# The last block of a three-stage kernel in seven products, and a second phase with new places

## What is computed

```python
# attention, per head: state = gamma*state + k v^T ; y = scale * q state
x = attn_out.reshape(3072, 512)
h = x @ w_in                               # 512 -> 2048
g = where(h >= 1, h, where(h <= -1, 0, (h + 1)**2 / 4))
x = g @ w_out                              # 2048 -> 512
h = x @ w_in2                              # 512 -> 1024
solu = h * softmax(h)
ln = (solu - mean(solu)) / sqrt(var(solu) + 1e-6) * g_ln
out = ln @ w_out2                          # 1024 -> 512
```

## Time and profile before

| | |
|---|---|
| three runs | 850.82, 851.32, 851.6 us; median 851.32 |
| profiled execution | 851.47 us, of which the span of the trace is 849.7 us |
| PE busy | 842.8 us, 99% of the span |
| DVE, ACT, POOL busy | 65%, 42%, 35% |
| granted PE clock | full in all 40 slices of the span |

### The profile page before, as it was taken

The page is one execution under the profiler, slowest core; times in us unless marked ns, Lnnn a source line. Parts: engine busy times, 40 slices in busy tenths (PEclk is TensorE's granted clock), DMA queues, the critical chain, the costliest instruction groups (busy, mean ns, idle before and its releaser), DMA issues.

```text
span 849.7 us, 14124 instructions
## 1 busy us (share of the span) xinstructions
PE 842.8 (99%) x5392; PEld 718.7 (85%) x5392; DVE 548.8 (65%) x1020; ACT 356.0 (42%) x557; POOL 293.6 (35%) x278
## 2 busy tenths in 40 slices
PE   8999999999999999999999999999999999999998
PEld 7788888888888888888988888888887888888886
DVE  5556567766754575545854563566888898898831
ACT  3444342323322243223422233256566766675642
POOL 2687555445323253324322222236441112221000
PEclk9999999999999999999999999999999999999999
DMA  9934358864443435443443404200165554456351
GB/s 338 386 113 143 125 174 305 259 204 149 150 134 129 139 122 161 146 133 123 135 148 124 125 26 149 100 25 25 51 217 170 167 165 150 149 186 181 117 175 61
DMA packets 75588, 129.14 MB, mean 152 GB/s; under 512 B 7552, under 2 KB 25984, under 8 KB 75520
## 3 DMA queue, kind: packets, MB, share of 16 engines
q1 hardware_dynamic: 74944, 127.71, 46.0%
q10 hardware_dynamic: 576, 0.52, 0.2%
HBM read 94.65 MB, written 33.55 MB: 151 GB/s over the span
## 4 chain that ended last, share of the span: by engine, by line
PE 94%; DMA 2%; DVE 1%; SPq 1%; issue 1%; POOL 0%; ACT 0%; DVEq 0%
PE acc L646 31%; PE h L550 19%; PE o_ps L1448 14%; PE p L1348 11%; PE h L616 10%; PE att L493 3%; PE att L504 2%; PE att L528 1%; PE att L518 1%; DMA z<-zq 1%; DMA q<-in_q 1%; DMA x_raw<-x2T 1%; PE acc L504 0%; PE h L633 0%; SPq L322 0%
## 5 line engine op out<-in xcount | busy, mean ns | idle before, releaser
L646 PE MATMUL acc<-g_hi,w 128*128 128x512 f32 x768 | 258.7, 398 | 0.0
L1122 POOL TENSOR_TENSOR g_lo<-g_raw,g_hi 128x512 fp32r<-128x512 f32 x96 | 130.9, 1364 | 312.4 <-ACT g_hi L690 312.4
L646 PEld LDWEIGHTS acc<-g_hi,w 128*128 128x128 f32 x768 | 144.1, 188 | 35.7 <-issue 3.4
L760 ACT ACTIVATE g_raw<-g_raw,half_bias 128x512 f32<-128x512 f32 x96 | 69.2, 721 | 234.4 <-DVE g_raw L972 234.4
L985 DVE TENSOR_TENSOR h<-h 128x256 f32<-128x256 f32 x192 | 81.1, 423 | 110.5 <-PE h L550 79.4
L646 PE MATMUL acc<-g_lo,w 128*128 128x512 f32 x384 | 150.1, 391 | 0.0
L690 ACT ACTIVATE g_hi<-g_raw 128x512 fp32r<-128x512 f32 x96 | 60.7, 632 | 86.6 <-DVE g_raw L977 86.6
L550 PE MATMUL h<-x_hi,s 128*128 128x256 f32 x512 | 93.7, 281 | 0.0
L972 DVE TENSOR_SCALAR g_raw<-h 128x512 f32<-128x512 f32 x96 | 52.1, 543 | 61.4 <-PE acc L646 59.7
L977 DVE TENSOR_TENSOR g_raw<-h,g_raw 128x512 f32<-128x512 f32 x96 | 68.2, 710 | 23.9 <-ACT g_raw L760 23.9
L550 PEld LDWEIGHTS h<-x_hi,s 128*128 128x128 f32 x512 | 81.0, 189 | 2.4
(11 more groups left out here) (140 smaller groups left out, 1491.4 us busy)
## 6 DMA issues: line engine op xcount, KB each, us to landing
s<-w_sums SPq DMA_DIRECT2D x128, 256.0 KB, 2.8
z<-zq SPq DMA_DIRECT2D x24, 512.0 KB, 2.8
zt<-z SPq DMA_DIRECT2D x92, 128.0 KB, 3.1
kT<-in_kT SPq DMA_DIRECT2D x24, 256.0 KB, 3.1
q<-in_q SPq DMA_DIRECT2D x24, 256.0 KB, 2.8
v<-in_v SPq DMA_DIRECT2D x24, 256.0 KB, 3.2
w_sums<-s_made SPq DMA_DIRECT2D x6, 1024.0 KB, 5.1
x2T<-y SPq DMA_DIRECT2D x24, 256.0 KB, 3.3
```

What stands on the lines that cost most here:

```text
L646: last = mm(acc[m][:, :], ww, gg[:, f % 2, :], start=f == 0 and t == 0, stop=f == FT1 - 1 and t == 2)
L760: nc.scalar.activation(gate[:, f % 2, :], gate[:, f % 2, :], ACT.Square, bias=half_bias[:, 0:1], scale=0.5).then_inc(sem["squared"], 1)
L1122: tt(g[1][:, f % 2, :], gate[:, f % 2, :], g[0][:, f % 2, :].bitcast(F32), ALU.subtract)\
```

## The change

Block 5 becomes the fifth block in seven products, for its first 14 pieces (7 pairs, `WHOLE` = 14); pieces 14 and 15 stay one by one. The order at the end of block 5 on PE is: up 14, down 12, up 15, down 13, and then the second phase, whose first pair is now P1, P2, P6, P7, P4, P5, P3 with nothing between P7 and P4, followed by down 14 and 15. The sums of w2_in move from DVE to POOL (at pairs 2 and 3). The preparation of ACT and DVE moves to the ends of pairs 3 to 6 and to the new `last_steps`; the four last low parts of w2_out on DVE now stand before the joins of the first pair. ACT's high parts of the second piece of x2 (x2_1 and its sums) move behind `copy_part(0)`. In the last block x has eight parts, since b12 is needed beside t1, and t1 gets a place of its own. In the second phase P1 of the fourth pair (n = 3) is issued ahead of down product 2. Tiles of the second phase get new addresses.

```diff
-SEVEN = range(1, BLOCKS - 1)
-LAST_Q = FPAIRS * len(SEVEN)
+SEVEN = range(1, BLOCKS)
+LAST = BLOCKS - 1
+WHOLE = FT1 - 2
+LAST_Q = FPAIRS * (len(SEVEN) - 1) + WHOLE // 2
+def pairs(blk):
+    return range(WHOLE // 2 if blk == LAST else FPAIRS)
+X_ORDER = (("t3", "b11", "b21", "t2", "t1", "b22", "t4"), ("b11", "b21", "t3", "t2", "t1", "b22", "t4", "b12"))
...
# SP
+                    if blk == LAST and p == 4:
+                        load_w2_out()
...
+                    if blk == LAST and p == 0:
+                        load_w2_in()
...
-                sp.wait_ge(sem["g_used"], FT1 * (BLOCKS - 1) + 8 + 2 * n)
+                sp.wait_ge(sem["g_used"], FT1 * LAST + 10 + 2 * n)
...
# PE
-                for p in range(FPAIRS):
+                for p in pairs(blk):
                     pair(blk, p)
-            dense(BLOCKS - 1)
+            for f in range(WHOLE, FT1):
+                up(LAST, f)
+                down(LAST, f - LAG)
...
# ACT
+            def prepare(p):
+                for kt in {3: (0, 1), 4: (2, 3)}.get(p, ()):
+                    w2_in_high(kt)
+                if p == 5:
+                    for i in range(3):
+                        w2_sum_high(i)
+                for piece in {5: (0, 1), 6: (2, 3)}.get(p, ()):
+                    w2_out_high(piece)
+
+            def last_steps():
+                square(LAST, WHOLE - 1)
+                high(LAST, WHOLE - 1)
+                x2_high(0)
+                x2_sum_high(0)
+                square(LAST, WHOLE)
+                high(LAST, WHOLE)
+                for piece in (4, 5):
+                    w2_out_high(piece)
+                square(LAST, WHOLE + 1)
+                high(LAST, WHOLE + 1)
+                for piece in (6, 7):
+                    w2_out_high(piece)
...
# DVE
+            def prepare(p):
+                for kt in {4: (0, 1), 5: (2, 3)}.get(p, ()):
+                    w2_in_low(kt)
+                if p == 6:
+                    for i in range(2):
+                        w2_sum_low(i)
+
+            def last_steps():
+                dve.wait_ge(sem["taken1"], 7 * LAST_Q)
+                clamp(LAST, WHOLE - 1)
+                larger(LAST, WHOLE - 1)
+                w2_sum_low(2)
+                dve.wait_ge(sem["gains"], 16)
+                for piece in range(2):
+                    w2_out_lo(piece)
+                clamp(LAST, WHOLE)
+                x2_low(0, "x2_0")
+                larger(LAST, WHOLE)
+                x2_low(1, "x2_sum0")
+                for piece in range(2, 4):
+                    w2_out_lo(piece)
+                clamp(LAST, WHOLE + 1)
+                larger(LAST, WHOLE + 1)
...
# POOL, in pair(blk, p), behind low(blk, f)
+                if blk == LAST and p in (2, 3):
+                    sums_of_w2(p - 2)
+                if blk == LAST and p == 6:
+                    sums_of_x2(0)
...
+            def last_steps():
+                for f in range(WHOLE - 1, FT1):
+                    low(LAST, f)
+                    if f == WHOLE:
+                        sums_of_x2(1)
...
# second phase, PE
-                    finish["pe_down"](FT1 - LAG - 1)
-                    finish["pe_up"]()
                     pe.wait_ge(sem["taken"], 1)
                     p4()
...
-                    p1()
+                    if n > 3:
+                        p1()
...
                 for s in DOWNS.get(n, ()):
+                    if s == 2:
+                        up_first(3)
                     down(s)
...
# second phase, ACT
             copy_part(0)
-            finish["act_square"]()
-            finish["act_high"]()
+            x2_high(1)
+            x2_sum_high(1)
             exponential(0, SECOND)
...
# second phase, DVE
+            for piece in range(4, FT2):
+                finish["dve_w2_out"](piece)
             join_p2(0)
             join_p6(0)
             join_p7(0)
-            for piece in range(4, FT2):
-                finish["dve_w2_out"](piece)
-            finish["dve_clamp"]()
             join_p4(0)
-            finish["dve_larger"]()
             join_p5(0)
             join_p3(0)
```

More of the change, by code:

```diff
@@ L220, in place @@
         split_in_place(f"x2_sum{n}", [P, 4, 2, P])
-    assert cursor[0] <= w_at + 10 * 8192
+    assert cursor[0] <= w_at + 12 * 8192
+    for name in ("h2", "e"):
+        plain(name, [P, 2, FF2])
+    assert cursor[0] <= w_at + 14 * 8192
+    plain("zq", [P, 2, P // SQ, FT2, SQ])
+    assert cursor[0] <= w_at + 15 * 8192
+    plain("zt", [P, 2, P // SQ, FT2, SQ])
+    zT = [[put(f"zT{n}_{part}", [P, FT2, P], F32R) for part in ("hi", "lo")] for n in (1, 2)]
+    assert cursor[0] <= y_at
+    cursor[0] = x3_at
+    plain("solu", [P, 2, FF2])
+    split("zT0", [P, FT2, P])
+    mem["zT1"], mem["zT2"] = zT
     zT_hi4 = cursor[0]
     cursor[0] += P * FT2 * 4
[L224 to L232, removed]
+    assert cursor[0] <= w_pair_at
     cursor[0] = g_at
@@ L650, in dense @@
             def dense(blk):
-                for f in range(steps(blk)):
-                    if blk == 0 and f == 0:
+                for f in range(FT1):
+                    if f == 0:
                         first_up()
@@ L767, in dense @@
             def dense(blk):
-                if blk - 1 in SEVEN:
-                    square(blk - 1, FT1 - 1)
-                    high(blk - 1, FT1 - 1)
-                for f in range(steps(blk)):
-                    change = f == FT1 - 1 and blk + 1 == SEVEN[0]
-                    if f == FT1 - 2 and blk + 1 == SEVEN[0]:
+                for f in range(FT1):
+                    change = f == FT1 - 1
+                    if f == FT1 - 2:
                         split_part(blk + 1, "t3")
@@ L801, in pair @@
                 f = 2 * p
-                more = blk + 1 in SEVEN and p == FPAIRS - 1
-                last = blk + 1 not in SEVEN and p == FPAIRS - 1
+                more = blk < LAST and p == FPAIRS - 1
                 if p == 1:
@@ L837, in _ @@
             for blk in SEVEN:
-                for p in range(FPAIRS):
+                for p in pairs(blk):
                     pair(blk, p)
-            dense(BLOCKS - 1)
-            finish["act_square"] = lambda: square(BLOCKS - 1, FT1 - 1)
-            finish["act_high"] = lambda: high(BLOCKS - 1, FT1 - 1)
+            last_steps()
+            finish["act_x2"] = (x2_high, x2_sum_high)
             finish["act_evacuate"] = lambda: evacuate(BLOCKS - 1)
@@ L1033, in pair @@
                         sums_low(q + AHEAD, n)
+                if blk == LAST:
+                    prepare(p)
             def dense(blk):
-                if blk - 1 in SEVEN:
-                    dve.wait_ge(sem["taken1"], 7 * LAST_Q)
-                    clamp(blk - 1, FT1 - 1)
-                    larger(blk - 1, FT1 - 1)
-                for f in range(steps(blk)):
-                    change = f == FT1 - 1 and blk + 1 == SEVEN[0]
-                    if blk < BLOCKS - 1:
-                        attention(blk + 1, 2 * f)
-                    if f == LAG - 1 and blk:
-                        evacuate(blk - 1)
+                for f in range(FT1):
+                    change = f == FT1 - 1
+                    attention(blk + 1, 2 * f)
                     if change:
@@ L1081, in _ @@
             for blk in SEVEN:
-                for p in range(FPAIRS):
+                for p in pairs(blk):
                     pair(blk, p)
-            dense(BLOCKS - 1)
+            last_steps()
             finish["dve_w2_out"] = w2_out_lo
-            finish["dve_clamp"] = lambda: clamp(BLOCKS - 1, FT1 - 1)
-            finish["dve_larger"] = lambda: larger(BLOCKS - 1, FT1 - 1)
             finish["dve_evacuate"] = lambda: evacuate(BLOCKS - 1)
@@ new lines, in dense @@
+            def dense(blk):
+                for f in range(FT1):
+                    attention(blk + 1, 2 * f)
+                    attention(blk + 1, 2 * f + 1)
+                    for name in {FT1 - 3: ("t3",), FT1 - 2: ("t1", "t2", "t4")}.get(f, ()):
+                        sum_of_x(blk + 1, name)
+                    low(blk, f)
+                    for piece in w_out_at(f):
+                        split_weights(piece)
+                    if f in PREPARE_AT:
+                        sums_of_weights(PREPARE_AT.index(f))
@@ L1790, in _ @@
             finish["pool_x2_lo"](1)
-            finish["pool_low"]()
             root(0, SECOND)
```

387 lines of the change are left out of this document (181 added, 206 removed).

## The result

| | before | changed |
|---|---|---|
| median | 851.07 us (850.44 to 851.6, 4 runs) | 858.48 us (857.71 to 860.11, 4 runs) |
| profiled execution, span of its trace | 851.47, 849.7 | 858.88, 857.1 |
| granted PE clock over the span | 1.0 | 0.998 |

The changed kernel is slower: ratio 1.0085, 95% interval 1.0072 to 1.0097, or +7.4 us. The forecast was 857.0. The page of the changed kernel, busy time, gives PE 846.3 us, against 842.8, and 10.8 us of the span without work, against 6.9.

The account below looks back on a forecast made before the run. PE, busy 99% of the span, was taken as the bound. Products -2.9, P1 ahead of down product 2 -1.1, late pairs +2.2 and block 5's end +7.4 gave +5.6: 857.0 us; range 848.8 to 861.0, the forecast's own 854 to 860.

Parts of the forecast that it names:

- Part 1: Block 5 to P1 of the second pair of tiles: fewer products, 99.54 us against 102.44, PE alone -2.9 us.
- Part 2: Second phase: P1 ahead of down product 2 fills its wait for zT_lo, -1.1 us.
- Part 3: Pairs of block 5: side engines' results come late at the first, third, fourth and after the fifth pair, +2.2 us in sum.
- The step on SP: Block 5 pairs: w2_out's eight loads ahead of two loads of sums cost nothing; without cover a pair would wait about 2 us.
- Part 4: End of block 5: DVE and POOL SBUF works add up, making PE late by 7.4 us (0.9 at least, 10 at most).
- Down product 13: End of block 5: g_lo of 13 behind POOL's sums of x2 and a DVE instruction, +0.7 us.
- P7: First pair of tiles: P7 waits for ACT's copy of P1, behind `clamp` of piece 15, and is 5.4 us late.
- P4: First pair of tiles: P4 waits until DVE has joined P2, behind four w_out_lo, 0.9 us more.
- rival C: Second phase's start: PE stands over 5 us, its clock falls from P7 to P3, some 2.7 us: 859.7 us, chance 0.12.
- a sign of being wrong: Start of the second phase: the granted clock falls below full in that slice (rival C).
- Rival A: End of block 5: DVE keeps ahead, P7 0.9 us late, P4 not at all: 849.4 us, chance 0.20.
- turning point: At `clamp` 15: the outcome turns to Rival A when DVE's backlog is under about 2 us.

Follow-up runs that it names:

- the first experiment: Against the changed kernel, ACT copies P1 out ahead of the gate of piece 15 and the last two w2_out high parts: 861.64 us.
- both edits: Against the changed kernel, ACT copies P1 ahead of the last gate and DVE joins ahead of w2_out low parts from piece 2 on: 860.31 us.

## Why the prediction was right, and where its steps were off

**Part 1, the products: right.** Pairs of block 5 without a wait last 10.45 us (forecast 10.49), and the single pieces 5.44. That makes 10.76 + 6 x 10.45 + 10.88 + 14.96 = 99.3 us without a wait from block 5 to the second pair of tiles, against 102.6 before: -3.3 for -2.9. Of the 0.4, 0.16 is a slip of the forecast: it took block 5's start (507.16) from the chain of waits and the end (609.60) from the timeline, where the start stands at 507.00. With the preparation spread the stretch took 101.22, that is with 1.9 us of waits in it.

**Part 2, P1 ahead of down product 2: right.** From down product 1 to 3 it takes 20.50 us against 21.65, so -1.15 (forecast -1.1), and undone it comes back.

**Part 3, the pairs: 2.2 forecast, 2.2 found, differently split.** Its terms were off by up to 0.4 us and balance by luck. The first pair takes 11.49 (+0.7 for +0.5), the fourth 11.18 (+0.7 for +0.6), the fifth 10.50 (0 for +0.4), the seventh 11.19 (+0.7 for +0.7). The fourth came by the steps of the forecast. POOL, pair 3, which starts at 540.63:

```profile
542.43 2.40 POOL L1214 TENSOR_TENSOR w_sum_raw<-w_in_raw 128x1024 f32<-128x1024 f32 x1
544.80 2.86 POOL L1216 TENSOR_TENSOR w_in_raw<-w_in_raw 128x1024 f32<-128x1024 f32 x1
547.62 1.28 POOL L1150 TENSOR_TENSOR g_lo<-g_raw,g_hi 128x512 fp32r<-128x512 f32 x1
...
558.12 1.30 POOL L1150 TENSOR_TENSOR g_lo<-g_raw,g_hi 128x512 fp32r<-128x512 f32 x1
```

`low` ends 8.3 after the pair's start, as forecast, and 7.7 was due. In pair 4 the same `low` ends at 559.42 and PE takes it at 559.52: the +0.4 there is 0, by 0.1 us. A further 0.3 lies at the end of block 4, whose last down product takes 3.03 us up to block 5 instead of 2.76; the forecast had not asked whether the border now costs there too. The step on SP held: no load of sums released a product.

**Part 4, the end of block 5: the mechanism right, its terms too large, and the clock not in it.** The forecast had 7.4 (0.7 and 0.4 ahead of P1, 5.4 at P7, 0.9 at P4). Found: 0 and 0.2 ahead of P1, 4.7 at P7, none at P4, and 1.7 from the clock, with 0.2 of small distances 6.8. E, the end of pair 6, is 583.95.
- Down product 13: `low` of 13 was put at E + 8.75 and ended at E + 8.0 (589.84 + 2.10), in time. The term was mis-sized.
- P7: `clamp` 15 was put at E + 16.8 and came at E + 15.4, P7 at E + 21.5 and came at E + 20.0. DVE's list took 16.6 us where the sum had 17.8, and began 0.15 earlier: adding the whole of POOL's SBUF time (6.3) to DVE's was too much by some 1.2 us. P1 was 0.9 early too, so P7 is 0.7 less late than forecast.
- P4: at full speed it would have been due 1.36 behind P7, at 605.33, and DVE read the joined maximum at 605.82. So the 0.9 would have been 0.5, and the slower clock hid it: P4 started at 606.70.
- The clock: rival C had its fall, over all from P7 to P3, at 2.7 us. It came, and cost 1.7, as full speed was back within ten matmuls. Here the forecast's choice between itself and C failed: it had put the fall at nothing, and named it as a sign of being wrong. The mechanism of part 4 stands, but the term for the clock was missing from it.

**Not in the forecast:** the place of zT (0.15 and 1.41, some 1.5 us), which the forecast took as free of cost, and start and border, 1.24 in this profile. From the forecast's +5.6: +2.8 for these two, -0.6 in part 4, -0.4 in part 1, makes the 7.4 of the trace. The sign and the place of the loss were right since the mechanism and its main terms held. That the number came as near as 1.5 us is in part luck: costs put at nothing (place, start and border, clock) make 4.5 us, and terms put too high in parts 4 and 1 make 2.7 the other way.

**Rival A** fell by its turning point: it needed a backlog of under 2 us at `clamp` 15, and 4.4 were found. The experiment with the preparation spread makes A's condition true: there the backlog is 1.2 us, and the time 849.79, where A had 849.4. So near a hit is chance, as orders and places differ there too.

## What to carry to other kernels

When products are taken from a saturated PE, the side engines' work in that stretch doesn't shrink with it: sum it between two deadlines, with DVE's and POOL's SBUF instructions added up and not laid side by side, before any order is written. If that sum is too large, an exchange of order only picks the place of the wait; start the work earlier instead. And look at new addresses as a part of the change: read the distance between matmul starts by buffer, not only the waits.

## What the runs showed of the hardware

- **The clock after a stall.** Idle for 4.57 us, PE got 0.50 for about 3 us, and ten matmuls cost 1.7 us more; the first experiment, idle for 7.4 us, shows the same distances of 0.43 behind its stall. The profiles with POOL's sums moved, idle for 3.0 us, and with the joins first, idle for 3.5, have a granted clock of 1.0 over the whole span. But the one with both edits fell to 0.50 behind 3.1 us of idle time, 1.2 us after PE had restarted, and seven distances of 0.43 us followed. So gaps of 3.0 to 3.5 us went both ways here.
- **Turns between DVE and POOL cost both sides.** Six w_out_lo of 0.66 took 8.85 us beside two subtractions of 128x1024 on POOL (2.70 and 2.84); a 128x512 `low` on POOL took 2.10 for 1.29. DVE's `clamp` of a joined tile in SBUF took 0.96 at 586.17, and 0.43 at 580.97.
- **Place in SBUF.** The stationary operand of a 128x512 matmul, read from offsets between 196160 and 216640 of a partition, stretched the distance of matmuls from 0.227 to 0.233 us, from down product 3 on in the tiles that lay there and in no others. No wait shows it, only the distances do.
